# Attention inside a dense TensorE stream: two pairs of pieces share a slot and a pair of PSUM banks, and the last block is cut in halves

## The reference

```
q_d, k_d, v_d = mean over groups of 4 positions            # coarse: 144 x 144 scores per head
out_up    = repeat(softmax(scale q_d k_d^T) v_d, 4)
out_local = softmax(where(|i - j| < 4, scale q k^T, -1e9)) v   # local: a band of 7 keys
x  = out_up + out_local                                     # (4, 576, 512)
x  = x + relu(layernorm(x) * g @ w_ch1) @ w_ch2              # 512 -> 2048 -> 512
xk, xr = mixes of x and of x one position earlier
out = sigmoid(xr @ w_r) * (relu(xk @ w_k)^2 @ w_v)          # 512 -> 1024 -> 512
```

## Time and profile before

| | |
|---|---|
| three runs | 776.99, 775.06, 776.60 us, median 776.6 |
| the profiled execution | 776.24 us, span 774.4 us |
| granted PE clock | 0.999 |
| PE busy | 752.2 us, 97% |
| DVE, ACT, POOL busy | 437.2, 275.8, 226.1 us |
| PE in the chain that ended last | 88% |

### The profile page before, as it was taken

How to read it: one execution, slowest core, us unless ns; L and a number is a source line. 1 busy time by engine, 2 the same in 40 slices (tenths; PEclk the granted TensorE clock), 3 DMA queues, 4 the chain that set the end, 5 groups by cost and what they waited for, 6 DMA issues and landing times.

```text
span 774.4 us, 15774 instructions
## 1 busy us (share of the span) xinstructions
PE 752.2 (97%) x6412; PEld 692.3 (89%) x6412; DVE 437.2 (56%) x811; ACT 275.8 (36%) x654; POOL 226.1 (29%) x261
## 2 busy tenths in 40 slices
PE   5799999999999999999999999999999999999997
PEld 4599989999999999999999999998888888888886
DVE  5867664444654354564353432466687676766655
ACT  5665432222223233222232231455433434333322
POOL 5167654134343223434323212004111111112101
PEclk9999999999999999999999999999999999999999
DMA  9892440220441021252011002722003001010010
GB/s 180 217 301 52 98 95 22 49 58 17 82 94 40 16 53 56 53 96 52 14 25 39 3 13 78 258 85 67 20 1 108 1 31 52 1 55 1 0 55 28
DMA packets 117960, 49.68 MB, mean 64 GB/s; under 512 B 96640, under 2 KB 106880, under 8 KB 117888
## 3 DMA queue, kind: packets, MB, share of 16 engines
q1 hardware_dynamic: 117888, 48.68, 24.7%
HBM read 39.20 MB, written 9.45 MB: 63 GB/s over the span
## 4 chain that ended last, share of the span: by engine, by line
PE 88%; DVE 3%; SPq 2%; ACT 2%; POOL 2%; issue 2%; DMA 1%; POOLq 0%; DVEq 0%
PE psH L981 24%; PE psY L998 24%; PE psH L1032 13%; PE psY L1051 12%; PE psA L1014 6%; PE psA L884 2%; PE psA L915 2%; SPq L542 1%; POOL x L763 1%; PE psA L895 1%; PE psA L860 1%; PE psA L832 1%; PE psA L845 1%; ACT prob L1125 1%; POOL rstd L758 1%
## 5 line engine op out<-in xcount | busy, mean ns | idle before, releaser
L1613 DVE SCALAR_TENSOR_TENSOR h_lo<-psH,h_hi 128x288 fp32r<-128x288 f32 x128 | 58.4, 456 | 204.6 <-ACT h_hi L1311 204.6
L981 PE MATMUL psH<-xc_hi,w_hi 128*128 128x288 f32 x512 | 154.9, 303 | 2.4 <-DVE xc_lo L1483 2.4
L998 PE MATMUL psY<-h_hi,w_hi 128*128 128x288 f32 x512 | 156.1, 305 | 0.1
L981 PE MATMUL psH<-xc_lo,w_hi 128*128 128x288 f32 x512 | 151.9, 297 | 0.0
L981 PE MATMUL psH<-xc_hi,w_lo 128*128 128x288 f32 x512 | 151.9, 297 | 0.0
L998 PE MATMUL psY<-h_lo,w_hi 128*128 128x288 f32 x512 | 150.8, 295 | 0.0
L998 PE MATMUL psY<-h_hi,w_lo 128*128 128x288 f32 x512 | 150.7, 294 | 0.0
L1311 ACT ACTIVATE h_hi<-psH 128x288 fp32r<-128x288 f32 x128 | 52.5, 410 | 224.0 <-PE psH L981 223.9
L806 POOL TENSOR_TENSOR relu_k<-relu_k 128x512 f32<-128x512 f32 (+1 forms) x40 | 39.0, 975 | 246.9 <-ACT relu_k L1274 246.9
L981 PEld LDWEIGHTS psH<-xc_hi,w_hi 128*128 128x128 f32 x512 | 97.0, 190 | 4.2 <-issue 3.2
L998 PEld LDWEIGHTS psY<-h_hi,w_hi 128*128 128x128 f32 x512 | 96.0, 187 | 4.6 <-issue 1.7
(11 more groups left out here) (174 smaller groups left out, 1347.0 us busy)
## 6 DMA issues: line engine op xcount, KB each, us to landing
w_raw<-in_moe_w_ch_dram SPq DMA_DIRECT2D x8, 1024.0 KB, 7.4
v_win<-in_v_dram SPq DMA_DIRECT2D x84, 56.0 KB
x_scratch<-x SPq DMA_DIRECT2D x8, 576.0 KB, 3.8
out_dram<-gate SPq DMA_DIRECT2D x18, 256.0 KB, 2.2
raw<-in_q_dram SPq DMA_DIRECT2D x112, 36.0 KB, 1.9
raw<-in_k_dram SPq DMA_DIRECT2D x96, 36.0 KB, 1.9
v_raw<-in_v_dram SPq DMA_DIRECT2D x12, 288.0 KB
x_sh<-x_scratch SPq DMA_DIRECT2D x3, 1026.0 KB, 5.7
```

Of the source, the lines that this page charges most:

```text
L981: ins = mm(psH[:, m % 2, 0:N], ws[a][:, kt, f * P:(f + 1) * P], xx[bb][:, kt], start=(kt == 0 and i == 0), stop=(kt == KT - 1 and i == 2))
L998: ins = mm(psY[:, d, 0:N], ws[a][:, f, d * P:(d + 1) * P], hs[bb][:, m % 2], start=(f == 0 and i == 0), stop=(f == NF1 - 1 and i == 2))
L1613: nc.vector.scalar_tensor_tensor(out=h_lo[:, m % 2], in0=psH[:, m % 2, 0:N], scalar=0.0, in1=h_hi[:, m % 2].bitcast(F32), op0=ALU.max, op1 ...
```

## The change

`LATER` gets another order. Window 0 of the local scores goes to slot 5, in front of the second coarse scores (moved from 4 to 5). Windows 1 and 2 go together in slot 11. The coarse values (from 13) and the local values of window 0 (from 16) both stand in slot 15; PT 0 goes from 14 to 13, PdT 0 from 7 to 8. So 13 slots with pieces become 11. The second piece of each pair does not wait for the bank; in `psA` the local scores and values lie behind the coarse ones, from column 288 (`OTHERS`) of each bank. Their readers wait for both pieces. PT 0 is copied into `y_tmp` and no longer into `probT`. `V_SUM` and `V_LOAD` move by one or two slots. The last flip of unit 2 goes a slot later.

At the end of the program the last step (`M_END`) is done by pieces of 128 positions, its square on DVE and not on POOL, and the last block's product and store by halves of 256 channels.

```diff
-    LATER = [(2, "Sd", 0), (4, "Sd", 1),
-             (7, "PdT", 0), (8, "S", 0), (10, "PdT", 1), (12, "S", 2), (13, "OD", 0),
-             (14, "PT", 0), (16, "AV", 0), (17, "PT", 1), (19, "PT", 2), (21, "AV", 1), (24, "M", 0)]
-    TOGETHER = {("S", 0): (0, 1), ("AV", 1): (1, 2), ("OD", 0): (0, 1)}
+    LATER = [(2, "Sd", 0), (5, "S", 0), (5, "Sd", 1), (8, "PdT", 0), (10, "PdT", 1), (11, "S", 1),
+             (13, "PT", 0), (15, "OD", 0), (15, "AV", 0), (17, "PT", 1), (19, "PT", 2), (21, "AV", 1), (24, "M", 0)]
+    TOGETHER = {("S", 1): (1, 2), ("AV", 1): (1, 2), ("OD", 0): (0, 1)}
+    OTHERS = 4 * GU
+    SECOND = [("Sd", 1), ("AV", 0)]
...
-    FLIPS_THIRD = [(-12, "k", 0, 0), (-10, "k", 0, 1), (-8, "k", 1, 0), (-4, "k", 1, 1), (-3, "q", 0, 0), (-2, "q", 0, 1)]
+    FLIPS_THIRD = [(-12, "k", 0, 0), (-10, "k", 0, 1), (-8, "k", 1, 0), (-4, "k", 1, 1), (-3, "q", 0, 0), (-1, "q", 0, 1)]
...
-        for g, (s, load) in enumerate(((14 + behind, 8), (20 + behind, 15 + behind), (27 + behind, 21 + behind), (39, 31))):
+        for g, (s, load) in enumerate(((16 + behind, 8), (22 + behind, 17 + behind), (28 + behind, 23 + behind), (39, 31))):
...
+        def shares(i):
+            return steps[i][1] >= 1 and (steps[i][0], steps[i][2]) in SECOND
...
-            if before:
+            if before and not shares(i):
+                if shares(before[-1]):
+                    wait_step_out(eng, before[-2])
                 wait_step_out(eng, before[-1])
...
+            if u and (kind, n) == ("PT", 0):
+                return y_tmp.rearrange("p a n -> p (a n)")
...
+            if u and (kind, n) in (("S", 0), ("AV", 0)):
+                at = OTHERS
...
+        def pieces(c, f):
+            n = tiles[c][1]
+            if c * NF2 + f < M_END:
+                return [(0, slice(0, n))]
+            return [(t, slice(t * P, (t + 1) * P)) for t in range(n // P)]
...
+                if u:
+                    act.wait_ge(av_done, count_of("AV", u, 0))
...
+                if u and n == 0:
+                    dve.wait_ge(sd_done, 2 * u + 2)
...
+                if m == M_END:
+                    dve.wait_ge(k_square, m)
+                    for i, at in pieces(c, f):
+                        r = relu_k[:, m % 2, at]
+                        dve.wait_ge(k_relu, m + i + 1)
+                        nc.vector.tensor_tensor(r, r, r, ALU.mult).then_inc(k_square, 1)
...
+                    for half in range(2):
+                        at = slice(half * (E // 2), (half + 1) * (E // 2))
+                        nc.vector.tensor_tensor(gate[:, t, at], gate[:, t, at], psY[:, t, at], ALU.mult).then_inc(out_ready, 1)
```

More of the change, by code:

```diff
@@ L139, in fused_kernel @@
     DVE_WORK = {("Sd", 0): [("top_d", 0, 0), ("sum_d", 0, 2)], ("Sd", 1): [("top_d", 1, 0), ("sum_d", 1, 2)],
-                ("S", 0): [("mask", 0, 0), ("mask", 1, 0), ("sum_p", 0, 3), ("sum_p", 1, 4)],
-                ("S", 2): [("mask", 2, 0), ("sum_p", 2, 3)],
+                ("S", 0): [("mask", 0, 0), ("sum_p", 0, 3)],
+                ("S", 1): [("mask", 1, 0), ("mask", 2, 0), ("sum_p", 1, 3), ("sum_p", 2, 4)],
                 ("AV", 0): [("x_out", 0, 0)], ("AV", 1): [("x_out", 1, 0), ("x_out", 2, 0), ("x_lo", 0, 2)],
@@ L675, in _ @@
                 for t in range(n // P):
-                    sp.wait_ge(out_ready, block_of(c, t) + 1)
-                    sp.dma_start(out[g0 + t * P:g0 + (t + 1) * P, :], gate[:, t, :]).then_inc(out_stored[t], 16)
+                    halves = 2 if block_of(c, t) + 1 == T // P else 1
+                    for half in range(halves):
+                        at = slice(half * (E // halves), (half + 1) * (E // halves))
+                        sp.wait_ge(out_ready, block_of(c, t) + half + 1)
+                        sp.dma_start(out[g0 + t * P:g0 + (t + 1) * P, at], gate[:, t, at]).then_inc(out_stored[t], 16)
             for t in range(CHUNKS):
-                sp.wait_ge(out_stored[t], 16 * sum(t < n // P for _, n in tiles))
+                last = 16 if t + 1 == tiles[-1][1] // P else 0
+                sp.wait_ge(out_stored[t], 16 * sum(t < n // P for _, n in tiles) + last)
         @block.gpsimd
@@ L803, in _ @@
                     m = c * NF2 + f
+                    if m == M_END:
+                        break
                     pool.wait_ge(k_relu, m + 1)
@@ L1042, in down_c @@
                 for t in range(tiles[c][1] // P):
+                    if m == M_END:
+                        pe.wait_ge(k_split, m + t + 1)
                     if f == 0:
@@ L1154, in pt_o @@
                 act.wait_ge(pt_done, w + 1)
-                if u >= 1:
+                if u >= 1 and n >= 1:
                     act.wait_ge(od_done, count_by("OD", u + 1))
-                    if n == 2:
-                        act.wait_ge(av_done, count_of("AV", u, 0))
-                elif n == 2:
+                elif u >= 2:
+                    act.wait_ge(x2_made, KT * (u - 1))
+                elif u == 0 and n == 2:
                     act.wait_ge(od_done, 1)
@@ L1273, in relu_c @@
                     act.wait_ge(k_split, m - 1)
-                nc.scalar.activation(relu_k[:, m % 2, 0:n], psH[:, m % 2, 0:n], ACT.Relu).then_inc(k_relu, 1)
+                for _, at in pieces(c, f):
+                    nc.scalar.activation(relu_k[:, m % 2, at], psH[:, m % 2, at], ACT.Relu).then_inc(k_relu, 1)
             def hi_k(c, f):
@@ L1278, in hi_k @@
                 m = c * NF2 + f
-                act.wait_ge(k_square, m + 1)
                 if m >= 2:
                     act.wait_ge(k_used, m - 1)
-                copy(kh_hi[:, m % 2, 0:n], relu_k[:, m % 2, 0:n]).then_inc(k_hi_ready, 1)
+                for i, at in pieces(c, f):
+                    act.wait_ge(k_square, m + i + 1)
+                    copy(kh_hi[:, m % 2, at], relu_k[:, m % 2, at]).then_inc(k_hi_ready, 1)
             turn_o("Tk", 0)
@@ L1509, in scale_y @@
                 dve.wait_ge(rs_in, 16 * (u + 1))
+                dve.wait_ge(av_done, count_of("AV", min(u + 1, NU - 1), 0))
                 for d in ds:
@@ L1635, in lo_k @@
                 m = c * NF2 + f
-                dve.wait_ge(k_hi_ready, m + 1)
-                nc.vector.tensor_tensor(kh_lo[:, m % 2, 0:n], relu_k[:, m % 2, 0:n], kh_hi[:, m % 2, 0:n].bitcast(F32),
-                                        ALU.subtract).then_inc(k_split, 1)
+                if m == M_END:
+                    dve.wait_ge(k_square, m)
+                    for i, at in pieces(c, f):
+                        r = relu_k[:, m % 2, at]
+                        dve.wait_ge(k_relu, m + i + 1)
+                        nc.vector.tensor_tensor(r, r, r, ALU.mult).then_inc(k_square, 1)
+                for i, at in pieces(c, f):
+                    dve.wait_ge(k_hi_ready, m + i + 1)
+                    nc.vector.tensor_tensor(kh_lo[:, m % 2, at], relu_k[:, m % 2, at], kh_hi[:, m % 2, at].bitcast(F32),
+                                            ALU.subtract).then_inc(k_split, 1)
             scale_y(NU - 1, (0, 1))
```

11 lines of the change are left out of this document (7 added, 4 removed).

## The result

| | before | changed |
|---|---|---|
| five runs each, median | 776.18 us (775.06 to 776.99) | 772.22 us (771.06 to 773.09) |
| ratio, 95% interval | | 0.9949 [0.9935, 0.9964] |
| profiled execution, span | 776.24, 774.4 us | 772.22, 770.2 us |

The account below looks back on a forecast made before the run. PE, busy 752.2 of 774.4 us, was taken as the bound. Gains of 2.65 + 3.1 + 0.4 + 0.65 less 0.1 make 6.7 us, so 776.24 - 6.7 = 769.5 us; range 767.3 to 772.8.

Parts of the forecast that it names:

- A: At the pairs: the gap between the pieces keeps the cold price, 0.10 us a pair, giving 771.2 us; chance 0.16.
- B: At PdT 0: mask and maximum delay the second exponentials, PE waits 0.4 us a unit, giving 772.3 us; chance 0.10.
- C: Units 1, 3, 5: v's third load over 3.5 us late, PE stops at first `down_b`; 778.8 us; chance 0.03.
- The wait of the second coarse scores: Second coarse scores on PE: their wait for ACT's exponentials of the first goes, gaining 2.65 us.
- Two pairs a unit: Two pieces share a slot twice in each of 7 units: 0.22 us a pair, 14 pairs, gaining 3.1 us.
- The flip of unit 2: Variance of unit 1: its wait for `sum_lo`, 1.06 us, goes, 0.65 comes back; gain 0.4 us, from -0.5 to 1.06.
- The end: Last step, product and store in smaller pieces: 0.6 - 0.15 + 0.2, gaining 0.65 us, from 0.45 to 0.95.
- New queues: Reordered work on DVE, ACT, POOL and SP: together -0.1 us, down to -2.
- (e): SP's list: the third load of v comes 8 DMAs later in units 3 and 5 too; about 0.5 us remains to `rstd`.
- PE's idle time falls by 2 us: Sign in the profile after: the prediction is wrong if PE's idle time has not fallen by 2 us.
- The gap between the pieces: Sign between a pair's pieces on PE: 0.13 us if the forecast is right, 0.26 if A.

Follow-up runs that it names:

- e6: e1's kernel with one pair undone: coarse values in slot 14, first local values in slot 15; 771.49 us, ratio 0.9942.
- e9: The kernel before with only the last flip of unit 2 one slot later (-2 to -1); 775.73 us, ratio 0.9995.
- e1: The changed kernel with v's third sum moved from slot 28 to 34, behind `add_y`, and the fourth sum and load later; 769.87 us, ratio 0.992.
- e8: e1's kernel with the last flip of unit 2 back in its old slot (-1 to -2); 770.84 us, ratio 0.993.
- e3: The kernel before with only the slots of v's sums and loads set to those of the changed kernel; 778.12 us, ratio 1.0024.
- e5: e1's kernel with POOL's `rstd` one slot later too, behind the four `add_y`; 768.73 us, ratio 0.9905.
- e4: The changed kernel with the second piece of both pairs one slot later (slots 6 and 16); 790.05 us, ratio 1.0182.
- e2: The changed kernel with v's third load at slot 22, not 23, and its second sum at 21, not 22; 775.48 us, ratio 0.9993.
- e11: The changed kernel with only POOL's `rstd` moved behind the four `add_y`, v's third sum left late; 769.34 us, ratio 0.9915.

## Why the prediction was right, and where it was wrong

The direction and the likeliest mechanism held; the time was 2.7 us above the forecast because one small term was mis-sized. That it still lies in the range is in part luck: the upper end, 772.8, was set by A and B, which did not happen, while C, whose mechanism did, was left out of the range. The terms, in the prediction's order:

1. *The wait of the second coarse scores*, 2.65 forecast. Right. In unit 3 the block ahead of them took 2.17 us before and its like 1.69 now: 0.48 a unit, 0.49 forecast.

2. *Two pairs a unit*, 3.1 forecast (0.22 a pair). Right. A clean period fell by 0.93 (61.60 to 60.67). Without 0.48 for the wait, and 0.20 for the pair that e6 measured by itself, 0.25 is left for the other, by subtraction and not by a run of its own. 7 x 0.45 = 3.15. The size was right for a partly wrong reason: the gap was thought to be a new cost that eats half of a free change of neighbours, and in fact the first piece keeps its old way out, 0.15 to 0.16 us from its last start where 0.13 or 0.26 were named. The rule of the Trainium skill (TensorEngine Tiling (Array Packing), Tiling Modes: a change of mode drains) fits the trace, in that the change from one piece's mode to the other's is no cheaper than that to a large matmul, 0.61 us in both rows of e6; if that is a drain, it was in the old price already.

3. *The flip of unit 2*, 0.4 forecast. By itself it is worth 0.17 (e9), and in e1's kernel nothing (e8). The step that failed is the first half, "its wait of 1.06 goes": in the new order 0.5 of it had gone without the flip (e8). What had halved it was not settled; that SP issues v's load after and not ahead of that `raw` fits, since e3 alone took 0.2 of it. The second half, that 0.65 comes back, was right in size (0.70 in e9), but of that 0.17 came back at the first `down_b` and 0.50 at the second coarse scores. In e1's kernel, where those have no wait, it came back at the first `down_b`; there it was POOL's order, since with `rstd` behind (e5) the two periods are 118.68 against e8's 119.23, and e8 had no long block at `down_b` for `rstd` to shorten.

4. *The end*, 0.65 forecast. Measured 0.44 - 0.07 = 0.37. The halves of the last product and store (0.2 - 0.15 = +0.05) cost 0.07: the product's part was 0.17, and the 0.2 for fewer bytes, read from a 36 KB and a 256 KB row, was 0.10. PE's part, 0.6, was 0.44: 0.18 of the wait stayed where 0.1 was left for it. Each of the first piece's four steps took 0.29 to 0.31 us, as forecast.

5. *New queues*, -0.1 forecast, down to -2. Measured -2.7: 0.14 in period 1-2, 1.88 in 3-4, 0.69 in 5-6, the difference of the changed kernel and e1. **This is the step that failed**: "(e) SP reaches the third load of v 8 DMAs later in units 3 and 5 too; about 0.5 us remains to `rstd`". In unit 3 the sum ended at 227.40, 2.2 us *after* `var_e`. The 0.5 was one number for three units and given without its working, and the count in front of it is half of what the list holds: the load went behind 16 DMAs, 8 of `v_win` and 8 of `raw`, as term 3 and rival C had it for unit 1. In the kernel before these 16 end at 223.0. A load issued there and landing 4.2 us later, with 2.0 us of sums behind it, lets `rstd` start near 229.2, an estimate from rows of e3 and of the chain above, and `var_e` was done at 228.04: it would have been 1.2 us late without any pair. e3, which has the list without the pairs, lost 1.9 us over the three units; the other 0.8 came with the pairs. So a step with 0.5 us to spare by the forecast had none, and a term put at 0.1 us was 2.7.

Of the rivals C had the right mechanism, by place and by engine, and a condition that was too coarse: it asked for 3.5 us of lateness in each of three units. `rstd` came 2.2 us late in unit 3, 0.75 in unit 5 and not at all in unit 1. Below the condition it does not cost nothing but takes part of the gain. Its counter-argument, "in unit 1 the load had 9 us and needed 4", was true of the before and of the unit where it hurt least. What made unit 1's block long was mostly term 3's second half: `var_e` behind the flip's sums (0.45 us, which e5 takes away). The other 0.34 is the time that `var_e` was held beside POOL's `vd`; e1 takes it away, and loses 0.18 of it again two blocks on. A and B did not happen; B's slack was 0.8 and not 1.1. With term 5 at its measured size the sum is 776.2 - 2.65 - 3.15 + 2.7 - 0.2 (term 3) - 0.37 = 772.5, against 772.2. The traces account for 3.5 us without the start, where the medians differ by 4.0; the rest is no more than the start varies by.

Of the signs named ahead, "PE's idle time falls by 2 us" was just missed (22.2 to 20.3, by the page), with 1.4 of new wait in it. The gap between the pieces was nearer to the forecast's 0.13 than to A's 0.26.

## What to carry to other kernels

When a change moves a load in the list of a queue that issues small DMAs without a pause, count the DMAs that now stand ahead of it, from the order in the trace and not from the slots in a table, and set them against the time that was spare. Here 16 of them were 9 us. Put work that waits for a transfer behind, not ahead of, what frees the bottleneck's buffers; in an in-order list that is a matter of one number. And when an engine's small instruction takes several times its usual length, look at what the other engines run at that moment before looking for a wait.

## What the runs showed of the hardware that was not expected

- A small `TENSOR_SCALAR` of DVE (`var_e`, `bias_d`; 0.17 us) that met an instruction of POOL lasted until 0.02 to 0.03 us after that one's end, up to 1.25 us (105 of 312 in the thirteen profiles; e4's rows show one). Four waits of PE in e4 are 1.1 us longer for it.
- After two stops of PE of 2.0 us and more, one in e2 and one in e4, its granted clock fell to 0.50 for some 3.3 us (in e4 only 1.35 us after PE had resumed), and large matmuls started every 0.24 us instead of every 0.13. After three other stops of that length in e4 it did not fall.
- The last store of 128 KB ended 2.38 us after its issue and that of 256 KB 2.48, so half the bytes were worth 0.10 us.
- Most DMA issues on SP take 0.4 to 0.5 us, but between 50 and 520 us of the changed kernel sixteen took 1.0 to 2.0 (in the kernel before, sixteen took 1.0 to 1.5). One of them stands ahead of the late load: in e3's section the row of 8 `v_win` took 4.64 us, where the same row took 3.65 before. There is one near the same place in e11 and e1 (214.73, 215.93; here 214.77); the cause is not known.
- The stretch up to the first variance varies by 1.9 us between executions of kernels that are alike there, about half of what this change gains. A comparison of two profiled spans has to leave it out.
